# Other rest slots, an earlier ranking step and another start order in a fused attention and two-MLP kernel

## The reference, cut to what matters

```
# attention: batch 4, heads 8, seq 768, head_dim 64; keys: 4 sinks + a window of 128
scores = q @ k.T / sqrt(64);  masked;  a = softmax(scores);  x = a @ v      # x: 3072 tokens x 512
# first MLP: d_model 512, d_ff 2048
h = x @ w_in;  g = h - tanh(h);  x2 = g @ w_out
# mixture of 8 experts, top 1: 512 -> 1024 -> 512
logits = x2 @ w_gate + modality_bias[modality_id];  e = argmax;  p = softmax(logits)[e]
out[t] = p * (relu(x2 @ w1[e]) @ w2[e])
```

## Time and profile before

| | us |
|---|---|
| median of 3 runs | 1080.92 |
| lowest, highest | 1075.41, 1086.34 |
| the profiled execution's own time | 1086.34 |
| its span in the profile | 1084.7 |

### The profile page before, as it was taken

The page is one execution under the profiler, slowest core; times in us unless marked ns, Lnnn a source line. Parts: engine busy times, 40 slices in busy tenths (PEclk is TensorE's granted clock), DMA queues, the critical chain, the costliest instruction groups (busy, mean ns, idle before and its releaser), DMA issues.

```text
span 1084.7 us, 24221 instructions
## 1 busy us (share of the span) xinstructions
PE 993.5 (92%) x7776; PEld 625.6 (58%) x7776; DVE 696.9 (64%) x2464; ACT 612.5 (56%) x1425; POOL 399.3 (37%) x462
## 2 busy tenths in 40 slices
PE   0668988999998999999999999999899999899996
PEld 0534544555565565555465556555487777677774
DVE  5687967668977867886886885646765334633331
ACT  2787866666767767767676676536422224522221
POOL 2789885412435312425331242011022222232322
PEclk9967999999999999999999999999999999999998
DMA  9843111421313331321141130041025111111111
GB/s 246 306 131 70 36 35 35 120 73 35 68 33 69 55 105 36 57 78 35 36 99 35 36 64 2 1 157 58 1 43 197 58 53 48 39 40 49 49 49 38
DMA packets 25165, 75.22 MB, mean 69 GB/s; under 512 B 10032, under 2 KB 10416, under 8 KB 23536
## 3 DMA queue, kind: packets, MB, share of 16 engines
q1 hardware_dynamic: 16176, 60.65, 21.4%
q0 software_dynamic: 5728, 13.43, 3.9%
q10 hardware_dynamic: 3168, 0.02, 0.1%
HBM read 60.23 MB, written 14.12 MB: 69 GB/s over the span
## 4 chain that ended last, share of the span: by engine, by line
PE 57%; DVE 18%; POOL 7%; issue 6%; ACT 6%; DMA 5%; DVEq 1%; SPq 0%; ACTq 0%; POOLq 0%
PE h_ps L742 14%; PE acc L798 13%; PE pt_ps L1829 9%; PE h_ps L1880 5%; PE acc L1880 4%; DVE qk_top L400 3%; DVE g_raw L763 2%; PE x_out L699 2%; PE pt_ps L637 2%; PE s_ps L567 2%; PE s_ps L849 2%; DMA qk_raw<-in_qk 2%; DVE g_lo L783 1%; DVE pt_lo L624 1%; ACT g_hi L773 1%
## 5 line engine op out<-in xcount | busy, mean ns | idle before, releaser
L798 PE MATMUL acc<-w_out_all,g_hi 128*128 128x512 f16 x768 | 228.8, 379 | 0.0
L742 PE MATMUL h_ps<-xt_hi,w_in_all 128*128 128x384 f16 x960 | 198.1, 329 | 15.2 <-DVE g_raw L763 14.7
L798 PE MATMUL acc<-w_out_all,g_lo 128*128 128x512 f16 x384 | 146.0, 380 | 9.8 <-DVE g_lo L783 7.8
L742 PEld LDWEIGHTS h_ps<-xt_hi,w_in_all 128*128 128x128 f16 x960 | 92.0, 98 | 85.6 <-DVE g_raw L763 19.3
L620 ACT ACTIVATE pt_hi<-pt_ps 128x256 f16<-128x256 f32 (+1 forms) x192 | 68.9, 359 | 102.9 <-PE pt_ps L637 102.6
L783 DVE SCALAR_TENSOR_TENSOR g_lo<-g_raw,batch_scale,g_hi 128x384 f16<-128x384 f32 x128 | 88.8, 694 | 48.2 <-ACT g_hi L773 46.8
L100 POOL TENSOR_TENSOR tick<-tick 1x1 f32<-1x1 f32 x83 | 15.8, 190 | 279.8 <-ACT y L1896 118.0
L451 POOL TENSOR_TENSOR q_stack<-qk_raw,q_stack 64x768 f16<-64x768 f32 x31 | 50.8, 1638 | 179.9 <-ACT q_stack L447 179.8
L798 PEld LDWEIGHTS acc<-w_out_all,g_hi 128*128 128x128 f16 x768 | 75.1, 98 | 70.3 <-issue 0.5
L773 ACT ACTIVATE g_hi<-g_raw,batch_scale 128x384 f16<-128x384 f32 x128 | 78.0, 609 | 40.2 <-DVE g_raw L763 39.7
L600 ACT ACTIVATE normed<-probs,row_sum 128x260 f32<-128x260 f32 (+1 forms) x192 | 92.9, 484 | 13.0 <-DVE row_sum L595 12.5
(11 more groups left out here) (310 smaller groups left out, 2109.1 us busy)
## 6 DMA issues: line engine op xcount, KB each, us to landing
qk_raw<-in_qk SPq DMA_DIRECT2D x62, 454.0 KB, 6.1
raw<-in_w SPq DMA_DIRECT2D x16, 512.0 KB, 7.5
v_raw<-in_v SPq DMA_DIRECT2D x4, 1536.0 KB, 10.2
x_tokens<-x SPq DMA_DIRECT2D x24, 256.0 KB, 6.5
w_in_all<-in_w_in SPq DMA_DIRECT2D x4, 1024.0 KB, 13.2
w_out_all<-in_w_out SPq DMA_DIRECT2D x4, 1024.0 KB, 12.0
x_tokens<-g_raw SPq DMA_DIRECT2D x1, 1024.0 KB, 13.6
qk_raw<-in_qk SPq DMA_DIRECT2D x2, 262.0 KB, 4.9
```

Source lines behind the costliest of these rows:

```text
L742: mm = eng.matmul(h_of(m, f), w16[0][:, f, x * DM + k * P:x * DM + (k + 1) * P], r[:, par, k, :], start=(i == 0), stop=(i == 3 * KD - 1))
L798: mm = eng.matmul(acc[t][:, :], l[f % 2][:, t * P:(t + 1) * P], w16[1][:, f, x * DM:(x + 1) * DM], start=(f == 0 and i == 0), stop=(f == N ...
```

## The change

The ranking step starts one slot earlier, at 25 in place of 26, except for g = NC-2. The rest slots of windows 1 and up are 1, 4, 6, 7, 19, 20, 22, 26 in place of 4, 5, 10, 11, 16, 17, 25, 26. At the start, the first two weight chunks and the sinks are issued ahead of `load_qk(2)`. All six `v_tops` and DVE's part of the spread move ahead of the first unit; PE's part of the spread and `v_scales` move from i = 1 to i = 0; and the first maximum of pair 1 moves from i = 1 to i = 0.

```diff
@@ -938,7 +938,7 @@
                 gate_logits(E, eng, g, (k - 7) // 6)
             if 20 <= k < 25:
                 gate_choose(E, eng, g, (k - 20,))
-            at = 27 if g == NC - 2 else 26
+            at = 27 if g == NC - 2 else 25
             if at <= k < at + 4:
                 gate_rank(E, eng, g, (k - at,))
 
@@ -1101,9 +1101,9 @@
                 load_qk(E, eng, 0)
                 load_v(E, eng, 0)
                 load_qk(E, eng, 1)
-                load_qk(E, eng, 2)
                 load_weights(E, eng, 0, range(2))
                 load_sinks(E, eng, 0)
+                load_qk(E, eng, 2)
                 load_weights(E, eng, 0, range(2, 4))
                 load_weights(E, eng, 1, range(1))
                 load_qk(E, eng, 3)
@@ -1115,14 +1115,16 @@
             qk_scales(E, eng, 0, 0)
             conv(E, eng, 0, 0, 0)
             conv(E, eng, 0, 0, 1)
-            v_tops(E, eng, 0, 0)
-            v_tops(E, eng, 0, 1)
+            for blk in range(NB2):
+                v_tops(E, eng, 0, blk)
+            if E == "dve":
+                spread(E, eng, 0)
             v_zero(E, eng, 0)
 
         def conversions(E, eng, i):
 
             for g in range(1, HP * NC):
-                tops = (1, 1, 1) if g == 1 else (6 * g - 10, 6 * g - 9, 6 * g - 8)
+                tops = (0, 1, 1) if g == 1 else (6 * g - 10, 6 * g - 9, 6 * g - 8)
                 splits = (3, 4) if g == 1 else (6 * g - 5, 6 * g - 3)
@@ -1137,12 +1139,8 @@
 
         def prepare_alone(E, eng, i):
 
-            if i < 2:
-                v_tops(E, eng, 0, 2 * i + 2)
-                v_tops(E, eng, 0, 2 * i + 3)
-            if i == 1:
-                if E in ("dve", "pe"):
-                    spread(E, eng, 0)
+            if i == 0:
+                spread("pe", eng, 0) if E == "pe" else None
                 v_scales(E, eng, 0)
                 for blk in range(TPC):
                     v_multiply(E, eng, 0, blk)
@@ -1257,7 +1255,7 @@
-                rest = k in ((13, 17, 19, 22, 30, 31) if w == 0 else (4, 5, 10, 11, 16, 17, 25, 26))
+                rest = k in ((13, 17, 19, 22, 30, 31) if w == 0 else (1, 4, 6, 7, 19, 20, 22, 26))
                 n = 10 ** 6 if rest else i
```

## The result

| us | before | after |
|---|---|---|
| median | 1080.97 (4 runs, 1075.41 to 1086.34) | **1092.97** (4 runs, 1088.64 to 1094.16) |
| ratio | | 1.0106 (95% interval 1.0066 to 1.0146) |
| the profiled execution | 1086.34, span 1084.7, clock 0.975 | 1094.88, span 1093.3, clock 0.977 |

The change makes the kernel 1.06% slower, some 12 us by the medians. That is 8 us above the forecast and just outside the wide range of 1071 to 1092. The two profiled executions differ by less, 8.5 us; why is told under "The profiled execution's own excess".

A forecast was written before the change was run, and what follows sets the result against it. The prediction took PE as the bound from window 1 on, with POOL fullest apart from PE in window 0. Windows +2.2 and start +1.7 gave +3.9 us on 1080.92, forecasting 1084.8 us; own range 1079 to 1090, wide range 1071 to 1092.

The forecast's parts named there:

- What bounds the kernel: From window 1 on PE is the bound, 87.57 of 89.50 us; a new slot order can only give back its idle time.
- The waits removed: PE's waits in windows 1 to 5, chiefly before slot 24, go: 3.15 us in odd windows, 6.60 in even, 9.75 in all.
- Term (1): Ranking before slot 25, windows 1 to 5: PE waits 1.3 us for DVE, whose scale step now falls in slot 23.
- the lock: Rival: in three odd windows POOL's L451 starts first and holds up DVE's L878, 6 us more, 1090.8 us; chance 0.08.
- Term (2): Windows 2 and 4, slot 22: choice part 2, meeting L451, and ACT's sinks' split add 1.1 us to the ranking wait.
- Term (3): Windows 2 and 4: scores wait for ACT's L839 in slots now carrying a unit, 1.2 us at 17, 0.4 at 11.
- The sum of the windows: Removed waits and the new waits in windows 1 to 5 together: +2.2 us.
- The start: Pair 2 lands behind the weights at 28.9, DVE asks at 27.2; the delay of 1.7 us passes to the end.
- The low clock: Rivals on PE's half-clock stretch near window 0: lasts longer, 1098 us, chance 0.10; ends earlier, 1078.8 us, chance 0.10.
- The sum: Whole kernel: windows +2.2 and start +1.7 make +3.9 us, a median of 1084.8 us; forecast's chance 0.40.

The follow-up runs named there:

- sinks_late: `choice_all_early` with sink_split in slot 26 instead of 22 in windows 2 and 4; 1082.00 us, ratio to the kernel before 1.0026.
- choice_all_early: The changed kernel with parts 1, 2 and 3 of gate_choose all in slot 21; 1084.44 us, ratio to the kernel before 1.0045.
- rank_26: The changed kernel with the ranking back at slot 26; 1083.62 us, ratio to the kernel before 1.0039.
- choice_early: The changed kernel with part 2 of gate_choose (L878, L879) moved from slot 22 to 21; 1089.67 us, ratio to the kernel before 1.0091.
- slots_only: The kernel before with only the new rest slots and the earlier ranking, start as before; 1087.05 us, ratio 1.0082.
- loads_only: The kernel before with only two weight chunks and the sinks loaded ahead of pair 2; 1082.79 us, ratio 1.0041.
- best_sinks_late: The kernel before with the new rest slots, gate_choose parts 1 to 3 in slot 21 and sink_split at 26 in windows 2 and 4; 1071.49 us, ratio 0.9921.
- run 99: A count, not a label: the unchanged kernel before was run 99 times beside the experiments; mean granted clock 0.972 to 0.988.

## Why the prediction was wrong, point by point

**What bounds the kernel, and the method.** Right: PE's idle time in windows 1 to 6 and the loads decide, and the two add up; the views show nothing else that the change moved.

**The waits removed (-9.75 us): this is the step that failed**, and in the odd windows alone. In windows 2 and 4 the 6.60 us went as said. In windows 1, 3 and 5 the three waits of 1.05 stayed and became 1.13. I put them to the units in slots 20 and 22 and counted L878 as 0.18 us, as it was in before's window 1. But it had begun there only 0.06 us ahead of L451, which the prediction itself says, without the number. Taking a unit out of the slots ahead changes which of them starts first, and then DVE loses 2.0 us. I saw this as a rival, at 6 us where it came to 4.6, and gave it 0.08, with no row that spoke for so low a chance. The Trainium skill's rule, in the section the prediction names, was a warning that should have moved it into the sum. Of two instructions that start within a few hundredths of each other and are both moved, either may be first.

**Term (1), 1.3 us at the ranking.** The mechanism is right, in windows 1 to 5 and nowhere else. Freed of the lock it measures 1.35 us in the odd windows, so its size was right too. In after it is 1.74, since the lock reaches slot 24 with 0.39.

**Term (2), 1.1 us more in windows 2 and 4.** The sum was right, 2.15 and 2.23 us in place of 2.4; the cause was the smaller half of what the prediction named. It is ACT's wait for POOL at the sinks' split, as `sinks_late` shows. The meeting with L451, which L878 had before and L881 has after, cost nothing by itself there, as `choice_all_early` shows.

**Term (3), the gate copies.** 0.56 us at slot 17 in place of 1.2, and 0.24 at slot 11 in place of 0.4. Two short waits that I had not named, 0.27 us for L600 before slot 16 and 0.33 before `mlp_in` at slot 2, make up most of the difference in both even windows.

**The sum of the windows.** +2.2 us forecast. PE's waits grew by 5.1 us. The lock is 4.6 us of it, and the other sizes together came out 1.7 us smaller than forecast, most of it term (3). The windows grew by 6.3; 1.2 us of that were in no wait I can name.

**The start, +1.7 us.** The mechanism, the place and the passing on to POOL and to the first `mlp_in` are right, and so was the estimate of the landing, 28.9 against a mean of 28.7 in seven executions. What was mis-sized is what it was held against: the time at which DVE asks for pair 2, 27.2 us, came from one execution, the slowest of three, in which v landed late. In the seven executions of the old order it is 25.8 on average, so the loss is about 3 us. That 27.2 was the latest could not be seen from one profile. That it was the slowest of three runs was written beside it, and the bound of +3 should have been the value.

**The profiled execution's own excess.** The 5.4 us by which before's profiled run lies above its median are in part this late start, and in part the expert stage: 299.3 us there, 294.2 to 297.4 in the fifteen other profiles. A half-clock spell of 3.4 us from 935.0 on, which only one other profile has (`choice_all_early`, with 297.4 us), is part of it. Neither belongs to the kernel, which is why the two profiled executions differ by 8.5 us and the medians by 12.0.

**The low clock.** Neither rival came in the profiled execution. The long stretch at half clock lasts 30.7 us in both kernels (from 64.6 us before, from 70.0 after). A short spell of 3.4 us moved. But the clock does vary between executions by more than the forecast's whole 3.9 us, and both profiles drew the long stretch at its longest; the last section has the numbers.

**The sum.** 3.9 us were forecast. The lock's 4.6 and 1.2 more at the start, less the 1.7 of the other sizes, give 8.0, and 9.2 with the 1.2 that I can't place; the medians differ by 12.0, with an interval of some 4 us to either side. So the account is complete within the noise and no closer; some of the rest may be the clock, which is lower in after's executions (last section).

## What to carry to other kernels

Where a small DVE instruction with two SBUF inputs and a long POOL instruction are released at about the same moment, price the meeting into the sum, and look for all such instructions behind that moment: moving the first one away only handed the lock to the next here. When a wait is to be removed by moving work away from it, list what is left on the late engine in the slots between; here 1.5 us of scale step, and a split that waits for POOL, were enough to build it up again one slot later. A moment read off one profile is one draw, and one that comes behind a load can be off by more than the effect; hold a late transfer against the fastest run you have, not against the slowest. A stage of one profile that differs by 2 or 3 us should be laid beside its granted clock before it is put to the change.

## What the hardware showed

**The lock is decided by hundredths of a microsecond.** L878 took 0.18 us where it began 0.06 ahead of L451 and 2.19 where it began 0.02 behind. L783, with two SBUF inputs and 0.62 us long otherwise, took 1.50 in after's window 1, begun at 211.09 with L451 running from 210.54 to 212.18. L400, with one input in SBUF, and L763, which reads its first input from PSUM, ran beside POOL's L451 at their usual lengths. In after L400 began at 279.66 and took 0.94 us, with L451 running from 279.10 to 280.75; in `choice_all_early` L763 began at 258.92 and took 0.62, with L451 from 258.36 to 260.54.

**Pair 2's two halves part.** They are issued 0.5 us apart and of equal size. In after the first landed at 26.5 and the second at 32.3, while the two chunks ahead of them had been issued by 7.3; chunk 1 landed as late as 27.4. In `rank_26` and `sinks_late`, with the same order, DVE's L400 started 5 us earlier. What makes these 5 us in some executions stays open.

**A half-clock spell can move to another window.** A spell here is a stretch in which PE was granted half its full clock. Before had one of 3.4 us from 525.4 us on, in window 4. After has it from 360.2, in window 2, right behind the 2.15 us wait, as its stretch shows (0.66 is the mean of both levels):

```profile
360.00:365.00 5.00, 4.93 (x24) 2.26 (x25) 2.65 (x15) 2.12 (x7) 0.68 (x1) 0.66 0.02 5
```

It costs about 1.7 us: windows 2 and 4 of `choice_all_early` wait alike and take 90.1 and 91.8 us, with the spell in the latter. It stood behind the 2.15 us wait of window 2 and not behind the 2.23 of window 4 after, the other way round in `choice_all_early`, and behind both in `choice_early`. With the waits of 0.96 and 1.05 us of `sinks_late` it doesn't come at all in either window. Over all sixteen profiles it stands in 6 of the 10 even windows with a wait of over 2.1 us, in 3 of the 14 with one of 1.82, and in none of the 8 with at most 1.3. So part of what a removed wait gives back is the clock: window 4 fell from 91.8 us in `choice_all_early` to 88.8 in `sinks_late`, for 1.18 us less waiting.

**The clock varies between executions more than the forecast effect.** The long half-clock stretch at the end of the first stage lasts 30.7 us in six of the sixteen profiles, before and after among them, and window 0 then takes 104.1 to 104.7 us. In `slots_only`, `loads_only` and `best_sinks_late` it lasts some 20.4 us and ends before window 0, and the spell of 3.4 us that before has at 173.8 is missing; window 0 then takes 100.9 to 101.2. That is the 100.9 in the first table. The kernel before was run 99 times beside the experiments: its mean granted clock goes from 0.972 to 0.988, and its time goes with it. The 16 executions at 0.984 or more have a median of 1075.1 us, the 35 at 0.976 or less one of 1081.5. Of the 99, 19 lie above 0.981. Of the 46 executions of the six kernels that have the new rest slots and the ranking at 25, after's eight included, none does. So these kernels seem to lose the faster executions as well; why isn't shown, since `sinks_late` is one of them and has no spell in windows 2 and 4.
